# Gates' roots and logarithms between chunks on ScalarE, copies of values and outputs on ScalarE, running products on later tiles

## What is computed

```python
mag = np.sqrt(a_re * a_re + a_im * a_im)
scale = np.minimum(mag, 0.999) / (mag + 1e-06)
for t in range(S):
    new_re = ar * S_re - ai * S_im
    new_im = ar * S_im + ai * S_re
    S_re, S_im = (new_re + kv, new_im)          # kv = outer(k[t], v[t])
    y[:, :, t] = np.einsum('bhd,bhde->bhe', q[:, :, t], S_re)
```

```python
scores = scale * (q @ k.transpose(0, 2, 1)); a = softmax(causal(scores))
out += mask[..., None] * w[:, :, kk:kk + 1] * (a @ v @ wo[e])
```

## Time and profile before

| | us |
|---|---|
| median of 3 runs (lowest, highest) | 847.19 (846.03, 847.77) |
| the profiled execution, its own time | 845.17 |
| its span, first to last instruction | 843.4 |
| TensorE, VectorE, ScalarE busy | 688.4, 631.4, 375.3 |
| mean granted clock of TensorE | 0.953 of 2.4 GHz |

### The profile page before, as it was taken

One profiled execution on the slowest core, in us unless ns is written; L12 is line 12 of the kernel. 1 busy time (PEld: TensorE's weight loads), 2 busy tenths in 40 slices (PEclk: granted clock), 3 DMA queues, 4 the chain that ended last, 5 costly groups with the idle time before them and its releaser, 6 DMA issues.

```text
span 843.4 us, 13053 instructions
## 1 busy us (share of the span) xinstructions
PE 688.4 (82%) x5160; PEld 516.5 (61%) x5160; DVE 631.4 (75%) x1306; ACT 375.3 (45%) x647; POOL 0.2 (0%) x4
## 2 busy tenths in 40 slices
PE   0025656989988779899988779899988899999998
PEld 0024545866656667776655668677655688776565
DVE  4999897797999568996979658996889555543463
ACT  6402255424555462435545562434555323432463
POOL 0000000000000000000000000000000000000000
PEclk9998759999999979999989989999999999999999
DMA  8375373100057322400056422400044331000001
GB/s 330 145 218 144 83 188 119 70 1 0 1 162 238 90 58 75 187 1 1 0 158 199 133 57 77 188 0 1 1 140 139 100 95 40 0 1 2 0 2 57
DMA packets 95836, 73.83 MB, mean 88 GB/s; under 512 B 10912, under 2 KB 87968, under 8 KB 95136
## 3 DMA queue, kind: packets, MB, share of 16 engines
q1 hardware_dynamic: 95776, 73.01, 28.2%
HBM read 49.34 MB, written 23.65 MB: 87 GB/s over the span
## 4 chain that ended last, share of the span: by engine, by line
PE 53%; DVE 33%; ACT 7%; issue 4%; DMA 1%; SPq 0%; DVEq 0%; ACTq 0%
PE wide L1324 8%; PE wide L1314 8%; PE wide L1353 6%; PE wide L1372 4%; PE bank L1324 4%; PE wide L1249 3%; PE bank L1423 3%; PE wide L1407 3%; DVE nmax L1022 3%; PE wide L1348 2%; DVE araw L920 2%; PE wide L1261 2%; PE bank L1431 2%; PE bank L1353 2%; DVE m L815 2%
## 5 line engine op out<-in xcount | busy, mean ns | idle before, releaser
L1314 PE MATMUL wide<-x_hi_lo,win_hi 128*128 128x384 f32 x384 | 110.2, 357 | 7.0 <-DVE x_hi_lo L938 7.0
L1324 PE MATMUL wide<-heads,wout 128*128 128x384 f32 x256 | 91.9, 503 | 9.3 <-DVE heads L980 9.3
L1314 PEld LDWEIGHTS wide<-x_hi_lo,win_hi 128*128 128x128 f32 x384 | 70.9, 191 | 11.6 <-issue 9.0
L637 ACT ACTIVATE xs<-wide 128x896 f32<-128x896 f32 x48 | 44.1, 918 | 71.7 <-PE wide L1407 71.7
L1022 DVE TENSOR_REDUCE nmax<-wide 128x1 f32<-128x768 f32 (+2 forms) x96 | 55.3, 617 | 27.3 <-PE wide L1381 27.2
L976 DVE SCALAR_TENSOR_TENSOR cv<-h,wconv,cv 128x768 f32<-128x768 f32 x64 | 64.9, 1014 | 13.1 <-ACT cv L596 11.5
L1324 PEld LDWEIGHTS wide<-heads,wout 128*128 128x128 f32 x256 | 48.9, 195 | 40.7 <-DVE heads L980 12.4
L1249 PE MATMUL wide<-heads 96*128 96x128 f32 x384 | 57.3, 311 | 18.3 <-DMA heads<-heads_dram 18.3
L1372 PE MATMUL wide<-attn 64*128 64x512 f32 (+3 forms) x256 | 66.9, 494 | 2.3 <-ACT attn L613 2.3
L591 ACT ACTIVATE h<-wide 128x384 f32<-128x384 f32 x64 | 30.5, 491 | 84.9 <-PE wide L1314 54.5
L1249 PEld LDWEIGHTS wide<-heads 96*128 96x128 f32 x384 | 53.2, 221 | 23.0 <-DMA heads<-heads_dram 19.0
(11 more groups left out here) (138 smaller groups left out, 1374.9 us busy)
## 6 DMA issues: line engine op xcount, KB each, us to landing
heads<-heads_dram SPq DMA_DIRECT2D x96, 192.0 KB, 3.5
araw<-a_in SPq DMA_DIRECT2D x12, 768.0 KB, 6.4
araw<-qk_in SPq DMA_DIRECT2D x12, 768.0 KB, 8.3
heads_dram<-m SPq DMA_DIRECT2D x24, 384.0 KB, 2.8
heads_dram<-araw SPq DMA_DIRECT2D x24, 384.0 KB, 3.0
v<-v_in SPq DMA_DIRECT2D x4, 1536.0 KB, 6.9
out_dram<-h SPq DMA_DIRECT2D x24, 192.0 KB, 2.0
wout<-w_out_t SPq DMA_DIRECT2D x1, 1536.0 KB, 12.2
```

The costliest lines, as they stand in the source:

```text
L637: nc.scalar.activation(probT[:, t % PROBT, :], wide[2][:, 0:KEYS], ACT.Copy).then_inc(s_pc, 1)
L1314: last = MM(low[u % 2][:, 0:NT], w[:, k, mt * P:(mt + 1) * P], xs[:, k, n * NT:(n + 1) * NT], start=(k == 0 and part == 0), stop=(k == KT ...
L1324: last = MM(mlp_bank[u][:, 0:NT], wout[:, mt, k * P:(k + 1) * P], hgate(mt)[:, n * NT:(n + 1) * NT], start=(mt == 0), stop=(mt == MT - 1))
```

## The change

Four things, in one edit. (1) Batches 1 and 2: of the three roots two go to the end of the batch before, and one pair of `ln` and `guess` goes to each of the first three chunks; `norm` and `write_w` start one chunk later, the last pair goes into MLP tile 1. In batch 0 unit 2's gates go from chunk 5 to chunks 3 and 4. (2) `copy_v` and `copy_o` go from VectorE to ScalarE, and `copy_k(b + 1, 0)` waits for the last transposed probabilities instead of the last expert outputs. (3) The head steps go to tiles 2 to 6, one fill out of the MLP to its end; `w_squares` stand between the copies of values. (4) In attention, `inverse`, `scale_qk`, `qk_products`, `decay`, `squares` and `gate_sumsq` stand at other t.

```diff
-CUM_AT = [0, 2, 4, 6, 8, 10, 11, 11, 11]
+CUM_AT = [0, 0, 0, 2, 4, 6, 8, 10, 10]
+assert CUM_AT[-1] == HEAD
 HS = 64
 LEAD = 32
-CUM_AT_FIRST = [0, 0, 0, 2, 5, 8, 10, 11, 11]
...
+            def copy_v(b, i):
+                act.wait_ge(s_p, len(PROJECTIONS) * b + i + 1)
+                src = projection_bank[PROJECTIONS[i][3]]
+                nc.scalar.activation(vx[:, i, :], src[:, 0:E * HD], ACT.Copy).then_inc(s_pv, 1)
+                nc.scalar.activation(logit[:, i, :], src[:, E * HD:E * HD + E], ACT.Copy).then_inc(s_pv, 1)
...
+            def copy_o(b, pair, side):
+
+                act.wait_ge(s_o[side], SLOTS // 2 * b + 2 * pair + 2)
+                if pair:
+                    act.wait_ge(s_f[side], PAIRS * b + pair)
+                nc.scalar.activation(oT[:, side, :], out_bank[side][:, 0:2 * P], ACT.Copy).then_inc(s_oe[side], 1)
...
@@ -648,22 +661,18 @@
                 for c in range(NC):
                     if c + 1 < GAINS:
                         copy_k(b, c + 1)
-                    if b and more and c == 0:
-                        for u in range(UNITS):
-                            magnitude(b + 1, u)
-                        exp_tables()
-                        for u in range(UNITS):
-                            ln(b + 1, u)
-                            guess(b + 1, u)
+                    if b and more and c < UNITS:
+                        if c == 0:
+                            magnitude(b + 1, UNITS - 1)
+                            exp_tables()
+                        ln(b + 1, c)
+                        guess(b + 1, c)
...
-                    if b == 0 and c == NC - 1:
+                    if b == 0 and c == 4:
                         magnitude(1, 2)
-                        exp_tables()
-                        ln(1, 2)
-                        guess(1, 2)
                     copy_x(b, c)
...
+                        if c == 3:
+                            squares(1, 2)
                         if c == 4:
-                            squares(1, 2)
+                            exp_tables()
+                            ln(1, 2)
+                            guess(1, 2)
...
-                    if more and mt == MT - 1:
-                        w_squares(b + 1, 0)
                 sigmoid(b, MT - 1)
                 copy_mlp(b)
                 exp_tables()
+                for i in range(NC):
+                    copy_v(b, i)
+                    if more and i in (2, 4):
+                        w_squares(b + 1, i // 2 - 1)
                 if more:
                     w_ln(b + 1, 0)
                     w_guess(b + 1, 0)
-                    w_squares(b + 1, 1)
-                    w_ln(b + 1, 1)
-                    w_guess(b + 1, 1)
                 for u in range(NC, FIRST_PAIR):
                     copy_projection(b, u)
                     if more and u == NC + 1:
                         w_squares(b + 1, 2)
+                    if more and u == NC + 2:
+                        w_ln(b + 1, 1)
+                        w_guess(b + 1, 1)
...
                     for side in range(2):
                         if t + 2 < SLOTS:
                             probs(b, t + 2, side)
+                    if t >= E and t % E < 2:
+                        copy_o(b, t // E - 1, t % E)
                     if t > E and t % E == 1:
                         copy_out(b, t // E - 1, 0)
                     if t > E and t % E == 3:
                         copy_out(b, t // E - 1, 1)
-                    if b + 2 < B and t in (8, 10):
-                        squares(b + 2, (t - 8) // 2)
+                    if b + 2 < B and t in (6, 9):
+                        squares(b + 2, t // 3 - 2)
                 if more:
 
-                    for side in range(2):
-                        act.wait_ge(s_o[side], SLOTS // 2 * (b + 1))
+                    act.wait_ge(s_pt, SLOTS * (b + 1))
                     copy_k(b + 1, 0)
+                if b + 2 < B:
+                    for u in range(2):
+                        magnitude(b + 2, u)
+                for side in range(2):
+                    copy_o(b, PAIRS - 1, side)
                 for side in range(2):
                     copy_out(b, PAIRS - 1, side)
                 if b + 2 < B:
...
-            def copy_v(b, i):
-                dve.wait_ge(s_p, len(PROJECTIONS) * b + i + 1)
-                src = projection_bank[PROJECTIONS[i][3]]
-                dve.tensor_copy(vx[:, i, :], src[:, 0:E * HD]).then_inc(s_pv, 1)
-                dve.tensor_copy(logit[:, i, :], src[:, E * HD:E * HD + E]).then_inc(s_pv, 1)
...
-            def copy_o(b, pair, side):
-
-                dve.wait_ge(s_o[side], SLOTS // 2 * b + 2 * pair + 2)
-                if pair:
-                    dve.wait_ge(s_f[side], PAIRS * b + pair)
-                dve.tensor_copy(oT[:, side, :], out_bank[side][:, 0:2 * P]).then_inc(s_oe[side], 1)
...
@@ -1065,22 +1073,19 @@
                         gate_sumsq(1, 0)
                         gate_sumsq(1, 1)
                         split_w_in()
+                    if b == 0 and c == 3:
                         norm(1, 0)
+                        gate_sumsq(1, 2)
+                    if b == 0 and c == 4:
                         write_w(1, 0)
-                    if b == 0 and c == 3:
-                        norm(1, 1)
-                    if b == 0 and c == 4:
-                        write_w(1, 1)
-                        gate_sumsq(1, 2)
-                    if b and more and c < NC - 1:
-                        (write_w if c % 2 else norm)(b + 1, c // 2)
+                    if b and more and 1 <= c < NC - 1:
+                        (norm if c % 2 else write_w)(b + 1, (c - 1) // 2)
                 x_low(b, NC - 1)
-                if b and more:
-                    write_w(b + 1, UNITS - 1)
-
-                at = CUM_AT if b else CUM_AT_FIRST
+                if more and b == 0:
+                    norm(1, 1)
+
                 for mt in range(MT):
-                    k0, k1 = at[mt], at[mt + 1]
+                    k0, k1 = CUM_AT[mt], CUM_AT[mt + 1]
                     if mt >= 1:
                         gate_h(b, mt - 1)
                     conv(b, mt, 1)
@@ -1090,34 +1095,33 @@
                     if more and k0 < k1:
                         cum_combine(b + 1, 0, UNITS, k0)
                         cum(b + 1, 0, UNITS, k0 + 1, k1)
-                    if b == 0 and mt == 1:
-                        norm(1, 2)
-                        write_w(1, 2)
+                    if b == 0 and mt == 0:
+                        write_w(1, 1)
+                    if more and mt == 1:
+                        norm(b + 1, UNITS - 1)
+                        write_w(b + 1, UNITS - 1)
                 gate_h(b, MT - 1)
                 if more:
+                    cum(b + 1, 0, UNITS, HEAD, HEAD + 2)
                     w_sumsq(b + 1, 0)
-                for i in range(NC):
-                    copy_v(b, i)
-                    if more and i == 0:
-                        cum(b + 1, 0, UNITS, HEAD + 1, HEAD + 2)
-                    if more and i == 3:
-                        w_sumsq(b + 1, 1)
-                        cum(b + 1, 0, UNITS, HEAD + 2, HEAD + 3)
+                    cum(b + 1, 0, UNITS, HEAD + 2, HEAD + 3)
+                    w_sumsq(b + 1, 1)
                 expert_gates(b)
                 if more:
                     inverse(b + 1, 0)
-                    w_sumsq(b + 1, 2)
                 expert_gates2(b)
                 if more:
-                    inverse(b + 1, 1)
+                    w_sumsq(b + 1, 2)
                     scale_qk(b + 1, 0)
                 for side in range(2):
                     row_max(b, 0, side)
                 if more:
-                    qk_products(b + 1, 0, 1)
+                    inverse(b + 1, 1)
                 row_sums(b, 0)
                 for side in range(2):
                     scale_probs(b, 0, side)
+                if more:
+                    qk_products(b + 1, 0, 1)
                 for side in range(2):
...
                     if more:
                         if t == 0:
                             qk_products(b + 1, 0, 0)
-                        if t == 2:
-                            scale_qk(b + 1, 1)
+                        if t == 1:
+                            inverse(b + 1, 2)
+                        if t in (2, 5):
+                            scale_qk(b + 1, t // 2)
                         if t in (3, 4):
                             qk_products(b + 1, 1, 4 - t)
-                        if t == 5:
-                            inverse(b + 1, 2)
-                        if t == 6:
-                            scale_qk(b + 1, 2)
-                        if t in (7, 8):
-                            qk_products(b + 1, 2, 8 - t)
-                        if t == 10:
+                        if t in (6, 7):
+                            qk_products(b + 1, 2, 7 - t)
+                        if t == 9:
```

(10 more changed lines are left out.)

## The result

The changed kernel takes 813.37 us (median of 4 runs, 810.38 to 814.85) against 847.48 us before (4 runs beside it, 846.03 to 850.03): ratio 0.959, 95% interval 0.955 to 0.963. The forecast was 815, with a range of 805 to 831. The profiled execution took 814.83 us with a span of 813.0 us.

The account below looks back on a forecast made before the run. TensorE was taken as the bound, busy 688 of 843.4 us, with gains only in its waits. Terms summed to 36.7 us, less half clock leaving 32: 813.2 profiled, 815 timed, range 805 to 831.

Parts of the forecast that it names:

- chunk stages, batches 1 and 2: Chunk 1's scores to first product's second half: keys' copy wait of 5.17 us goes; 10.6 and 8.1 us off.
- batch 0, start of the product's second half: End of batch 0's chunks: product resumes at 141.4 instead of 146.29, 4.9 us sooner.
- three boundaries: Between batches: keys' copy no longer waits for expert outputs, so 1.12 us go at each, 3.4 us in all.
- MLP with projections, batches 0, 1, 2: Running products moved to later tiles take 5.1, 0.7 and 1.9 us off the MLPs; projections worth 0.
- attention, batches 0 to 3: VectorE steps at other t: batch 0 loses 0.8 us, batches 1 and 2 gain 2.4 and 0.7, batch 3 pays 0.3.
- half clock: TensorE at 1.2 GHz after remaining waits: 1 us a batch in attention, 3 in all, plus 1.7 for tile 6.
- the 36.4 forecast: Chunk stage of batches 1 and 2: 36.4 us each, against batch 3's 35.5, at clock 1.00.
- Chunk 5's outputs end at about 139.4: Batch 0: after these outputs, copy (0.85) and x_low (0.9) follow until 141.2, and the product resumes at 141.4.
- Tile 6: MLP: the last two running-product steps make TensorE wait 1.9 us there, 5.78 us gate to gate against 3.87.
- 1.7 us of half clock that I had set aside behind tile 6: MLP: half clock after the tile 6 wait, seen with three chances and taken once, 1.7 us.
- Copies at nothing: Projections: value copies moved to ScalarE, 0.4 us taken per 256-column copy, fit its time; worth 0.
- Sum 7.6: Attention: listed waits, including 0.75 us at t=10, said to total 7.6 us over batch 3's 40.35, giving 48.0.

Follow-up runs that it names:

- (1): Changed kernel with the three logarithms and exponentials of batches 1 and 2 together in chunk 0 again, two roots staying in the batch before: 819.28 us, ratio 0.967.
- (2): Kernel before with only the second and third logarithm and exponential spread over later chunks in batches 1 and 2, all roots in chunk 0: 837.43 us, ratio 0.987.
- (12): The changed kernel itself, unaltered, timed and profiled a second time on another chip: 811.30 us, ratio 0.959.
- (6): Changed kernel with batch 0's norm of unit 0 one chunk later and its write one chunk after that: 817.54 us, ratio 0.966.
- (10): Changed kernel with w_o product and output copy first, no running-product steps in tile 6, batch 0's sum of squares, norm and write behind chunk 5's mask: 801.99 us, ratio 0.946.
- (8): Changed kernel with the copy of the next batch's first keys waiting for the last expert outputs again: 824.35 us, ratio 0.973.
- (7): Changed kernel with the last two running-product steps moved from MLP tile 6 to behind the last gated tile: 807.73 us, ratio 0.955.
- (3): Changed kernel with running products, first fill, and batches 1 and 2's norm and write placed as in the kernel before: 819.62 us, ratio 0.966.
- (4): Changed kernel with the copies of values and expert outputs on VectorE again, at the places of the kernel before: 813.81 us, ratio 0.959.

## Why the prediction was right, and where its terms were off

Each term of the sum, in us taken off, forecast and measured by the windows of both kernels:

| step | forecast | measured |
|---|---|---|
| chunk stages, batches 1 and 2 | 10.6, 8.1 | 10.1, 6.6 |
| batch 0, start of the product's second half | 4.9 | 2.8 |
| three boundaries | 3.4 | 3.5 |
| MLP with projections, batches 0, 1, 2 | 5.1, 0.7, 1.9 | 5.05, 0.4, 1.7 |
| attention, batches 0 to 3 | -0.8, 2.4, 0.7, -0.3 | -1.7, 3.0, -1.0, -0.2 |
| end | 0 | 0.1 |
| sum | 36.7, less 4.7 for half clock: 32 | 30.4 |

The measured terms hold the half clock where it fell. The mechanisms of the chunk stage, the boundary and the MLP are shown by experiments; that the total of 815 came within 1.6 us of the measured one is luck in part, because terms missed both ways, as the points say. The new order within attention and the move of batch 0's gates weren't undone alone; their terms rest on the windows and rows of both kernels. Point by point:

- **Chunk stage.** The mechanism is shown from both sides: the block back costs 3.9 us a stage, 2.3 of it wait (1), the spreading alone gives 6.6 and 4.1 (2). Batch 1's 36.85 us are the 36.4 forecast but for 0.4; batch 2 has 1.0 more by clock. The forecast that clock would be 1.00 held in one of two.
- **Batch 0.** In the profile the product is 2.1 us later than forecast: "Chunk 5's outputs end at about 139.4", and they ended at 141.3. The order is not to blame, and the step holds at full clock. From the end of chunk 4's outputs to the product it took 11.8 us before and 8.3 in this profile, with half clock behind the 2.76 us wait, but 6.9 in the second profile of the same kernel (12), where the product started at 140.97; that is the 4.9 us of the forecast. The rest, 0.7 us, is that chunk 4's outputs ended later here than before (135.17, not 134.50). What holds chunk 5's mask is read in (6): a sum of squares that waits for ScalarE's squares, beside the norm. To move it, with norm and write, behind the mask loses 2.4 us (10).
- **Boundary.** Right, and (8) shows why it was close: the roots fit only because the keys' copy no longer waits. With the wait back a boundary with roots takes 4.6 to 5.5 us more than in the changed kernel, and 3.4 to 4.3 more than in the kernel before.
- **MLP.** Tile 6 waited 1.54 us (1.9 forecast); (7) takes it away and 0.3 us with it, (3) gives back batch 0's term. The 1.7 us of half clock that I had set aside behind tile 6 was in none of its three stages, all at 1.00.
- **Copies at nothing.** Right (4). ScalarE's copy of 256 columns takes 0.39 us, forecast 0.4. The 5.0 us a batch that the prediction gives for them, twelve copies of 0.42, is off in its count: half the value copies have 4 columns, and six copies of expert outputs come with them. VectorE lost 4.4 us a batch.
- **Attention.** The waits came as listed (1.55, 1.81 for 1.7, 1.32, 0.24, 0.67 for 0.6, 1.06 for 0.9), but for the last, 0.16 us and not 0.75. At full clock the stage is 47.36 us, 0.6 below the 48.0 forecast. Most of this is a slip: the waits that the prediction lists add up to 7.1 us and not to its "Sum 7.6". Counted from batch 3's 40.56 they came to 6.8. Two of three attentions had half clock that cost 1.6 and 1.7 us (48.92 - 47.36; 48.88 less batch 2's 47.18 at clock 1.00 in experiment 8), where I had 1.0 in each of three.

So the half clock, 4.7 us forecast, stood partly in the wrong places and came to 5.8 in this execution: 1.5 in batch 0's last outputs (3.34 us from 137.93 to the product at 141.27, 1.89 in batch 1 at full clock), 1.0 in batch 2's chunks, 3.3 in attention. 36.7 less 5.8 is 30.9, and 30.4 were measured.

## What to carry over

Cut the program at the same instructions into stages, take the stage without the extra work as the measure, and cost an edit by who is last there: moving 4 us of copies a batch off the busier engine was worth nothing, moving 3.4 us of ScalarE's work out from in front of one copy was worth 4 us twice, 2.3 of them wait. Before an order on one engine is turned round, look at what stands behind the delayed instruction on the next engine: the same edit gave 4 us with an output copy behind the exponentials and 8 us without. Count an instruction's start from an event shortly before it, and look at the clock between: from the start of the program, one order seemed 1.2 us better where it was 1.2 us worse (10). And where one wait is shortened, look for the next one.

## What the hardware showed

After a wait of some 1.5 to 2.9 us TensorE's granted clock falls to the 1.2 GHz level for a few us in some places and not in others. In two executions of the same program the wait of 2.76 or 2.77 us in batch 0 was followed once by half clock and once by full clock (8.3 and 6.9 us to the product), and in the kernel before a wait of 3.25 us at the same place, before 137.75, by full clock. The chunk-5 wait of batch 1, 1.89 us in the changed kernel, was followed by full clock, and the same wait, 1.90 us, in experiment 6 by half clock (36.85 and 37.87 us for the stage). Attention with the same order, batches 0, 1, 2, in us (clock):

```
changed kernel  48.92 (0.97)  47.36 (1.00)  48.88 (0.93)
again           48.98 (0.97)  47.35 (1.00)  49.05 (0.93)
block back      48.97 (0.97)  47.35 (1.00)  47.18 (0.96)
products back   47.34 (1.00)  47.34 (0.96)  48.64 (0.93)
norm later      48.88 (0.93)  48.98 (0.93)  48.88 (0.93)
keys wait       48.97 (0.97)  48.87 (0.93)  47.18 (1.00)
tile 6 empty    47.35 (0.96)  49.19 (0.93)  47.16 (1.00)
```

It costs 1.5 to 1.9 us or nothing. At 0.96 the slower matmuls only used up the wait that follows: the second wait, 1.81 us at full clock, was 0.19 us, and full clock was back behind it. Where half clock lasted on behind the second wait (0.25 to 0.90 us left of it), or began there, it cost time. The wait of 1.54 us in tile 6, between long products, was followed by full clock in all three batches of all eight executions that have it. Experiment 6 was 4 us above the changed kernel in the medians, and its order explains 0.5 to 1.9 us of that, so differences of this size between orders aren't the orders' merit unless the windows show it in waits. What decides whether the clock falls at a given wait stays open.
